# All four blocks of the second batch form their up-projection from seven products

## The chip, the cores and the metric

The kernel runs on one core of a Trainium2 chip. The metric is the time of one execution in microseconds (us) on the device. Before the change it is 642.26 us, the median of three runs (642.01 to 642.44).

## What is computed

Three layers follow each other. Only the first feed-forward layer matters here.

```python
# attention: 2 batches x 8 heads, 576 positions, head size 64
x = (pooled attention repeated 4 times) + (attention in a band of +-3 positions)
x = x.transpose(0, 2, 1, 3).reshape(1152, 512)
# layer 1: 512 -> 2048 -> 512
h = x @ w_in
g = where(h > 0, h, exp(min(h, 0)) - 1)        # ELU
x = g @ w_out
# layer 2: 4 experts of 512 -> 1024 -> 512 with gates from domain_probs
```

Every float32 matrix product is made of three products on TensorE: each operand is split into a rounded part ("hi") and the rest ("lo"), and hi x hi, hi x lo and lo x hi are added up in PSUM. A split costs one copy on ScalarE (hi) and one subtraction (lo), on GpSimd for weights and on VectorE for activations.

## The kernel before

**Order of the work.** Attention goes by pairs of heads, u = 0 to 7; pairs 0 to 3 belong to batch 0, pairs 4 to 7 to batch 1. Layer 1 goes by blocks of 512 of the 2048 hidden units, four for each batch, numbered w = 0 to 7. Each engine has its own program, written out by hand, and waits on semaphores of the others. Nothing is reordered.

Blocks w = 0 to 3 (batch 0) are "mixed": `mixed_block1` runs 16 groups g of 12 matmuls with 288 columns (8 up-projections, 8 down-projections), and between them attention for pair u = w + 4 of batch 1. VectorE's `add_outputs` puts the output of the pair into `y_acc` (the raw x of batch 1), after the y addition of group 14. ScalarE's and VectorE's `split_x` then make `x_hi` and `x_lo` of it, in group 15.

Block w = 4, the first of batch 1, is plain: 16 groups of 12 matmuls, of which the first two are opened by `open_groups` in an order that starts with the x chunks that are ready first.

Blocks w = 5 to 7 are `block7`. Their up-projection is a 2 x 2 block product formed from seven products instead of eight (Winograd's form of Strassen's scheme): 7 x 2 x 6 = 84 matmuls, and 96 for the down-projection. The products stand in this order on TensorE, two PSUM banks each (p = 0, 1): P1 (weights and tokens as they are), P6 (weight sum S2 by token sum T2), P2, P5 (S1 by T1), P7 (tokens of the quadrant that T3 replaced), P4 (by T4), P3 (S4). They are joined by VectorE's `sum_u2`, `sum_w`, `sum_c22`, `sum_c21` and `sum_c12`; P4 waits for `sum_c22`, since it adds onto a bank that `sum_c22` reads. Between these sums lies the ELU of each finished part: ScalarE `exp_part` (Relu, Exp), VectorE `max_part`, ScalarE `hi_part`, VectorE `lo_part`.

**The token sums** T1 to T4 of batch 1 are made once: raw by VectorE's `add_x`, hi by ScalarE's `xt_hi`, lo by VectorE's `xt_lo`. Before the change this lies beside the 16 groups of the plain block w = 4. **The weight sums** of a block are made once for each block: raw by GpSimd's `add_ws` (4 instructions), hi by ScalarE's `split_ws`, lo by GpSimd's `split_ws` (7 instructions with the plain weights); for w = 5 this lies beside the plain block too.

Of the kernel before, what the change touches and what calls it, by code (L numbers as in the profile page):

```python
# [14 lines left out]
FACTOR = 4  # L15
# [47 lines left out]
BLOCKS7 = 3  # L63
# [14 lines left out]
T2_, T1_, T4_, T3_ = range(4)  # L78
T_RAW = (0, 1, 3)
# [11 lines left out]
OPEN = (4, 2)  # L91
# [21 lines left out]
def program(nc, q, k, v, w_in, w_out, probs, w1, w2, out):  # L113
# [12 lines left out]
    with ExitStack() as ctx:  # L126
# [30 lines left out]
        def input_set(spare):  # L157
# [6 lines left out]
        own_set = (sb1("q_in", [LT, NLT, 2 * HD])[:], sb1("k_in", [LT, NLT, 2 * HD])[:],  # L164
                   sb1("v_in", [PT, 4, FACTOR * HD])[:], sb1("v_win", [2 * WIN, CHUNKS, 2, HD])[:])
# [18 lines left out]
        x_sum = sb1("x_sum", [128, SEQ])  # L184
# [33 lines left out]
        def xt_raw(t):  # L218

            return h_spare2[:, t, 0:SEQ].rearrange("p (k n) -> p k n", k=2)  # L220
# [174 lines left out]
        def _(pe):  # L395
# [189 lines left out]
            def mixed_block1(i, u):  # L585

                for g in range(GROUPS1):
                    if not isinstance(i, int) or g >= OPEN[0]:
# [23 lines left out]
            def block7(w):  # L612
# [251 lines left out]
        def _(act):  # L864
# [67 lines left out]
            def group1(w, b, g, between=(), next_wa=True, this_wb=True):  # L932
                if g < UP1:
                    elu_parts(w, g)
                for step, *where in between:
                    step(*where)
                if 1 <= g <= UP1:
                    elu_hi(w, b, g - 1)
                if this_wb and g < FC - 1:
                    split_wb(w, g)  # L940
                if this_wb and g == FC - 2:
                    split_wb(w, FC - 1)
                if next_wa and g >= UP1 and g < UP1 + KC:
                    split_wa(w + 1, g - UP1, groups_before1(w) + UP1)

            def split_ws(w, n):

                v = w - FIRST7
                raw = s_raw1 if isinstance(w, int) and w < 2 * BLOCKS1 else s_raw
                act.wait_ge(wa_loaded, 16 * (w + 1))  # L950
                if n in (0, 1, 3, 4):
                    c = n if n < 2 else n - 1
                    act.wait_ge(s_raw_ready, 4 * v + 3)
                    nc.scalar.copy(wa_hi[:, c, :], wa_raw[:, c, :]).then_inc(wa_hi_ready, 1)  # L954
                else:
                    q = {2: S2, 5: S1, 6: S4}[n]
                    act.wait_ge(s_raw_ready, 4 * v + 4 if q == S4 else 4 * v + 3)
                    nc.scalar.copy(s_hi[:, q], raw[:, q]).then_inc(s_hi_ready, 1)

            def xt_hi(t):  # L960

                act.wait_ge(xt_raw_ready, {T1_: 1, T3_: 2, T2_: 3, T4_: 4}[t])
# [3 lines left out]
            def block7(w):  # L966
# [186 lines left out]
            for g in range(UP1 + 1):
                group1(BLOCKS1, 1, g, next_wa=False)
            split_ws(FIRST7, 0)
            split_ws(FIRST7, 1)
            split_ws(FIRST7, 2)
            xt_hi(T2_)
            split_ws(FIRST7, 3)
            split_ws(FIRST7, 4)  # L1160
            xt_hi(T1_)
            split_ws(FIRST7, 5)
            split_ws(FIRST7, 6)
            xt_hi(T4_)
            xt_hi(T3_)
            block7(FIRST7)
# [13 lines left out]
        def _(dve):  # L1180
# [109 lines left out]
            def add_x():  # L1290

                dve.wait_ge(out_free, OUT_CREDIT + 2 * PAIRS)
                nc.vector.tensor_tensor(xt_raw(T1_), x_quad(0, 1), x_quad(0, 0), ALU.subtract).then_inc(xt_raw_ready, 1)
                nc.vector.tensor_tensor(xt_raw(T3_), x_quad(1, 1), x_quad(0, 1), ALU.subtract).then_inc(xt_raw_ready, 1)
                dve.wait_ge(xt_raw_ready, 1)
                nc.vector.tensor_tensor(xt_raw(T2_), x_quad(1, 1), xt_raw(T1_), ALU.subtract).then_inc(xt_raw_ready, 1)
                dve.wait_ge(xt_raw_ready, 3)
                nc.vector.tensor_tensor(xt_raw(T4_), x_quad(1, 0), xt_raw(T2_), ALU.subtract).then_inc(xt_raw_ready, 1)
# [8 lines left out]
            def block7(w, beside):  # L1307
# [244 lines left out]
            add_x()
            lows = {12: [(xt_lo, 1, T2_)], 13: [(xt_lo, 2, T1_)], 14: [(xt_lo, 3, T4_)], 15: [(xt_lo, 4, T3_)]}
            for g in range(GROUPS1):
                group1(BLOCKS1, 1, g, lows.get(g, ()), first=True)
# [5 lines left out]
            block7(FIRST7, token_sums)  # L1561
# [21 lines left out]
            block7(FIRST7 + 1, gates_and_zeros)  # L1583
# [7 lines left out]
            block7(FIRST7 + 2, last_zeros)  # L1591
# [12 lines left out]
        def _(pool):  # L1604
            def sum_v(u):
# [3 lines left out]
                if not isinstance(u, int):  # L1609
# [113 lines left out]
            with pool.Fori(0, BLOCKS1) as i:  # L1723
# [13 lines left out]
            split_y(0, range(3))  # L1737
# [3 lines left out]
            split_ws(FIRST7 + 2, s_raw1)  # L1741
            split_y(0, range(3, Y_PARTS))
# [36 lines left out]
```

## Time and profile before

| | |
|---|---|
| median of the runs | 642.26 us |
| the profiled execution | 643.81 us |
| its span (first to last instruction) | 642.0 us |
| TensorE busy | 632.8 us (99%) |
| VectorE, ScalarE, GpSimd busy | 349.4, 283.4, 322.6 us |
| granted TensorE clock | 1.0 of full speed |

The chain that ended last is 94% TensorE, 3% VectorE, 2% ScalarE and 1% DMA. Rows below name engines as PE (TensorE matmul), PEld (its weight load), DVE (VectorE), ACT (ScalarE), POOL (GpSimd). A matmul is issued while the one before still drains, so rows of a matmul overlap: the step from start to start is its price, not its duration. The same holds, less strongly, for the other engines.

### The profile page before, as it was taken

Reading aid. Unit: us, or ns where it says so; the run is one execution under the profiler, and the core shown is the slowest. Engines: PE = TensorE matmul, PEld = TensorE weight load, DVE = VectorE, ACT = ScalarE, POOL = GpSimd, SP = SyncE. Lnnn points to the kernel's source line nnn. Section 1 sums busy time; section 2 is a strip of 40 time slices with the busy share of each in tenths; the row PEclk is TensorE's granted clock in tenths of the full one; section 3 lists DMA queues with packets and bytes.
Section 4 is the critical chain, followed back from the end, with each engine's and each line's share of the span. In section 5 each row is a group of like instructions: output and inputs, shape, how many; then the busy total and the mean of one; then the engine's idle time right before and its main releaser. Section 6 shows DMA issues by size and latency. Waiting matters only on the chain.

```text
span 642.0 us, 13095 instructions
## 1 busy us (share of the span) xinstructions
PE 632.8 (99%) x4775; PEld 584.8 (91%) x4775; DVE 349.4 (54%) x764; ACT 283.4 (44%) x786; POOL 322.6 (50%) x278
## 2 busy tenths in 40 slices
PE   8989999999999999999999999999999999999997
PEld 5779999999999999999899899899899899989986
DVE  4977454555567787673454364355265355355352
ACT  4888474747558578453152062152152142242210
POOL 3684545454497999887247056065064164160200
PEclk9999999999999999999999999999999999999999
DMA  9974525142241123103022021011012022020012
GB/s 169 185 195 135 137 72 141 65 105 65 67 131 67 65 80 117 66 27 107 0 58 75 2 65 65 0 65 65 0 65 65 0 65 65 0 66 2 0 50 98
DMA packets 51491, 46.10 MB, mean 72 GB/s; under 512 B 31616, under 2 KB 33920, under 8 KB 51456
## 3 DMA queue, kind: packets, MB, share of 16 engines
q1 hardware_dynamic: 50272, 45.34, 25.4%
q8 instruction: 21, 0.34, 0.2%
q10 hardware_dynamic: 1184, 0.30, 0.2%
q14 instruction: 14, 0.11, 0.1%
HBM read 43.27 MB, written 2.36 MB: 71 GB/s over the span
## 4 chain that ended last, share of the span: by engine, by line
PE 94%; DVE 3%; ACT 2%; DMA 1%; issue 0%; SPq 0%
PE psum L533 16%; PE psum L534 16%; PE psum L535 16%; PE psum L604 11%; PE psum L608 11%; PE psum L606 11%; PE psum L674 2%; PE psum L672 2%; PE psum L673 2%; PE psum L462 1%; DVE neg_max L1216 1%; PE psum L439 1%; DMA q_in<-in_q 1%; PE psum L525 1%; ACT attn L884 1%; PE psum L579 1%
## 5 line engine op out<-in xcount | busy, mean ns | idle before, releaser
L1630 POOL TENSOR_TENSOR wb_lo<-wb_raw,wb_hi 128x512 fp32r<-128x512 f32 x64 | 81.8, 1297 | 179.9 <-ACT wb_hi L913 179.7
L1440 DVE SCALAR_TENSOR_TENSOR o_acc<-psum,gate_now,o_acc 128x512 f32<-128x512 f32 x72 | 54.0, 751 | 126.0 <-PE psum L535 125.7
L535 PE MATMUL psum<-wb_hi,h_lo 128*128 128x512 f32 x288 | 112.3, 390 | 0.0
L534 PE MATMUL psum<-wb_lo,h_hi 128*128 128x512 f32 x288 | 112.2, 390 | 0.0
L533 PE MATMUL psum<-wb_hi,h_hi 128*128 128x512 f32 x288 | 112.0, 389 | 0.0
L1023 ACT ACTIVATE h_hi<-psum 128x320 fp32r<-128x320 f32 (+1 forms) x128 | 52.5, 412 | 87.3 <-DVE psum L1412 40.3
L1630 POOL TENSOR_TENSOR wa_lo<-wa_raw,wa_hi 128x512 fp32r<-128x512 f32 x60 | 77.5, 1317 | 16.8 <-ACT wa_hi L954 16.8
L1029 ACT COPY sums<-psum 128x256 f32<-128x256 f32 (+1 forms) x32 | 12.8, 400 | 155.1 <-PE psum L608 155.1
L608 PE MATMUL psum<-x_hi,wa_lo 128*128 128x256 f32 (+2 forms) x228 | 67.4, 296 | 0.0
L606 PE MATMUL psum<-x_lo,wa_hi 128*128 128x256 f32 (+2 forms) x228 | 67.3, 295 | 0.0
L604 PE MATMUL psum<-x_hi,wa_hi 128*128 128x256 f32 (+2 forms) x228 | 67.2, 295 | 0.0
L535 PEld LDWEIGHTS psum<-wb_hi,h_lo 128*128 128x128 f32 x288 | 54.1, 188 | 11.3
L1394 DVE SCALAR_TENSOR_TENSOR h_lo<-psum,h_hi 128x320 fp32r<-128x320 f32 (+1 forms) x128 | 54.9, 450 | 17.1 <-ACT h_hi L1023 17.0
L533 PEld LDWEIGHTS psum<-wb_hi,h_hi 128*128 128x128 f32 x288 | 54.1, 188 | 10.9
L534 PEld LDWEIGHTS psum<-wb_lo,h_hi 128*128 128x128 f32 x288 | 54.1, 188 | 10.8
L533 PE MATMUL psum<-h_hi,wb_hi 128*128 128x288 f32 x160 | 48.9, 306 | 0.1
L534 PE MATMUL psum<-h_lo,wb_hi 128*128 128x288 f32 x160 | 47.1, 294 | 0.0
L535 PE MATMUL psum<-h_hi,wb_lo 128*128 128x288 f32 x160 | 47.1, 294 | 0.0
L606 PE MATMUL psum<-t_lo,s_hi 128*128 128x320 f32 (+2 forms) x152 | 44.9, 295 | 0.0
L608 PE MATMUL psum<-t_hi,s_lo 128*128 128x320 f32 (+2 forms) x152 | 44.8, 295 | 0.0
L604 PE MATMUL psum<-t_hi,s_hi 128*128 128x320 f32 (+2 forms) x152 | 44.8, 295 | 0.0
L604 PEld LDWEIGHTS psum<-x_hi,wa_hi 128*128 128x128 f32 x228 | 43.0, 189 | 0.6
(192 smaller groups left out, 1667.1 us busy)
## 6 DMA issues: line engine op xcount, KB each, us to landing
wa_raw<-in_moe_w_in SPq DMA_DIRECT2D x8, 1024.0 KB, 5.3
wb_raw<-in_moe_w_out SPq DMA_DIRECT2D x8, 1024.0 KB, 5.2
wa_raw<-in_moe_w SPq DMA_DIRECT2D x8, 1024.0 KB, 5.0
wb_raw<-in_moe_w SPq DMA_DIRECT2D x8, 1024.0 KB, 5.1
out<-o_acc SPq DMA_DIRECT2D x9, 256.0 KB, 2.0
v_win<-in_v SPq DMA_DIRECT2D x20, 80.0 KB, 3.6
q_in<-in_q SPq DMA_DIRECT2D x10, 144.0 KB, 4.6
v_in<-in_v SPq DMA_DIRECT2D x5, 288.0 KB
```

The costliest lines, as they stand in the source:

```text
L533: nc.tensor.matmul(bank_cols, w_hi(n), x_hi_(n), start=(n == 0), stop=False)
L534: nc.tensor.matmul(bank_cols, w_hi(n), x_lo_(n), start=False, stop=False)
L535: last = nc.tensor.matmul(bank_cols, w_lo(n), x_hi_(n), start=False, stop=(n == chunks - 1))
L604: nc.tensor.matmul(bank, w_op[0][:, k, :], x_op[0][:, k, :], start=(start and k == 0), stop=False, skip_group_check=True)
L606: nc.tensor.matmul(bank, w_op[0][:, k, :], x_op[1][:, k, :], start=False, stop=False, skip_group_check=True)
L608: last = nc.tensor.matmul(bank, w_op[1][:, k, :], x_op[0][:, k, :], start=False, stop=(stop and k == 1), skip_group_check=True)
L672: nc.tensor.matmul(to, wb_hi[:, f, cols], h_hi[:, f, t], start=(f == 0), stop=False)
L673: nc.tensor.matmul(to, wb_hi[:, f, cols], h_lo[:, f, t], start=False, stop=False)
L1023: nc.scalar.activation(h_hi[:, 2 * fh + p, t0 + width * th:t0 + width * (th + 1)], psum[:, bank[p], 0:width], ACT.Relu).then_inc(h_hi_read ...
L1394: nc.vector.scalar_tensor_tensor(h_lo[at], bank(banks, p), 0.0, h_hi[at].bitcast(F32), ALU.max, ALU.subtract).then_inc(h_lo_ready, 1)
L1440: nc.vector.scalar_tensor_tensor(o_acc[:, m, :], psum[:, DOWN2_BANKS[(MT * half + m) % 2], :], gate_now[:, m:m + 1], o_acc[:, m, :], ALU.m ...
L1630: nc.gpsimd.tensor_tensor(lo[:, c, :], raw[:, c, :], hi[:, c, :].bitcast(F32), ALU.subtract).then_inc(lo_ready, 1)
```

## The change

`block7` now serves all four blocks of batch 1, w = 4 to 7 (`FIRST7` goes from 5 to 4). The plain block w = 4 with its `open_groups` start is gone.

- The weight sums of w = 4 are made in the last mixed block: GpSimd's `add_ws` comes behind its `split_wb(3)` and ahead of the three `normalise` of pair 7, `split_ws` behind them; ScalarE's seven `split_ws` take the place of the four `split_wa`, in groups 8 to 14.
- The token sums move too. VectorE makes T1 in group 12 of the last mixed block, the first half of T2 in group 13, the second half behind the y addition of group 15. T3, the last `x_lo` and T4 come inside block w = 4, and so do all `xt_hi` and `xt_lo`.
- The raw token sums lie in `o_acc`, `s_hi` and `s_lo` before `t_hi` and `t_lo` in memory, and waits for that are added.
- The additions into `y_acc` of w = 4 are copies, as in the plain block before. What the blocks w = 5 to 7 do beside their products stays with the same distance to the end.

```diff
-BLOCKS7 = 3
+BLOCKS7 = BLOCKS1
 # TensorE
-            for k in range(KC):
-                open_groups(BLOCKS1, 1, k, *range(OPEN[1]))
-            for g in range(OPEN[1], GROUPS1):
-                group1(BLOCKS1, 1, g)
+            pe.wait_ge(out_free, 2 * PAIRS + OUT_CREDIT)
+            pe.wait_ge(x_lo_ready, KC + 2)
             with pe.Fori(FIRST7, 2 * BLOCKS1) as w:
                 block7(w)
 # TensorE, block7, ahead of P2 and of P7, P4
+                pe.wait_ge(x_lo_ready, 2 * KC)
...
-                pe.wait_ge(xt_lo_ready, 4)
+                pe.wait_ge(xt_lo_ready, 3)
...
+                pe.wait_ge(xt_lo_ready, 4)
 # ScalarE, group1 of the last mixed block
+                if not next_wa and g >= UP1 and g < UP1 + KC + 3:
+                    split_ws(w + 1, g - UP1)
 # ScalarE, block7
+                if sums_of_x:
+                    xt_hi(T2_)
+                    xt_hi(T1_)
                 copy_p1(0)
-                split_wb(w, 0)
+                if not sums_of_x:
+                    split_wb(w, 0)
                 copy_p1(1)
+                if sums_of_x:
+                    xt_hi(T3_)
+                    xt_hi(T4_)
+                    split_wb(w, 0)
                 split_wb(w, 1)
                 split_wb(w, 2)
                 split_wb(w, 3)
                 exp_part(0, BANK_A, p2_done, 0)
 # VectorE, block7
+                if first:
+                    xt_lo(1, T2_)
+                    xt_lo(2, T1_)
+                    add_x(4)
+                    split_x(PAIRS - 1, 1, BLOCKS1 - 1)
+                    add_x(5)
                 sum_u2(0)
                 sum_u2(1)
+                if first:
+                    xt_lo(3, T3_)
                 max_part(0, BANK_A)
                 sum_w(0)
+                if first:
+                    xt_lo(4, T4_)
                 max_part(1, BANK_A)
 # VectorE, last mixed block
+                    12: [(add_x, 0)] if last else [],
+                    13: [(add_x, 2)] if last else [],
                     14: [(add_outputs, u, MIXED, i)],
-                    15: [(split_x, u, 1, i)],
+                    15: [(add_x, 3)] if last else [(split_x, u, 1, i)],
 # GpSimd
-            with pool.Fori(0, BLOCKS1) as i:
+            with pool.Fori(0, BLOCKS1 - 1) as i:
...
+            sum_v(PAIRS - 1)
+            split_wb(BLOCKS1 - 1)
             add_ws(FIRST7, s_raw1)
+            for j in range(3):
+                normalise(PAIRS - 1, j)
             split_ws(FIRST7, s_raw1)
             split_wb(FIRST7)
```

## Rows read from the trace of the kernel before

**Rows 1.** The page: busy time, share of the span, instructions of TensorE.

```profile
PE 632.8 (99%) x4775; PEld 584.8 (91%) x4775; DVE 349.4 (54%) x764; ACT 283.4 (44%) x786; POOL 322.6 (50%) x278
```

**Rows 2.** Windows, blocks w = 4 and w = 5: length, each engine's busy time, clock, DMA.

```profile
166.01:191.81 25.80, 25.70 (x194) 25.47 (x193) 16.74 (x32) 17.38 (x40) 20.08 (x15) 1.00 0.25 79
191.81:215.90 24.09, 24.09 (x183) 23.86 (x181) 19.79 (x40) 16.98 (x40) 18.67 (x14) 1.00 0.16 57
```

**Rows 3.** Timeline of TensorE (start, duration, instruction): P1, P2, P7's end, P4 of w = 5.

```profile
191.81 0.29 PE L604 MATMUL psum<-x_hi,wa_hi 128*128 128x288 f32 x1
...
194.97 0.29 PE L604 MATMUL psum<-x_hi,wa_hi 128*128 128x288 f32 x1
...
199.60 0.29 PE L608 MATMUL psum<-x_hi,wa_lo 128*128 128x288 f32 x1
199.88 0.40 PE L604 MATMUL psum<-t_hi,wa_hi 128*128 128x288 f32 x1
```

**Rows 4.** Timeline of VectorE where the last mixed block ends.

```profile
164.61 0.46 DVE L1285 TENSOR_TENSOR y_acc<-psum,y_acc 128x288 f32<-128x288 f32 x1 [2.72 <-PE psum L535]
164.98 0.81 DVE L1248 TENSOR_TENSOR y_acc<-psum,o_pooled 128x288 f32 x2
166.21 0.46 DVE L1285 TENSOR_TENSOR y_acc<-psum,y_acc 128x288 f32<-128x288 f32 x1 [0.41 <-PE psum L535]
...
167.43 0.75 DVE L1293 TENSOR_TENSOR h_spare<-y_acc 128x576 f32<-128x576 f32 x1
168.10 0.75 DVE L1294 TENSOR_TENSOR h_spare<-y_acc 128x576 f32<-128x576 f32 x1
```

**Rows 5.** Timeline of VectorE: a lo part of token sums with GpSimd busy, and idle.

```profile
189.19 1.22 DVE L1304 TENSOR_TENSOR t_lo<-h_spare,t_hi 128x576 fp32r<-128x576 f32 x1
...
192.46 0.74 DVE L1304 TENSOR_TENSOR x_lo<-h_spare,x_hi 128x576 fp32r<-128x576 f32 x1
```

**Rows 6.** Timeline of ScalarE: x split, token sums, weight splits and first ELU of w = 5.

```profile
165.94 0.68 ACT L903 CAST x_hi<-y_acc  x1 [2.81 <-DVE y_acc L1248]
...
185.80 0.67 ACT L964 CAST t_hi<-h_spare 128x576 fp32r<-128x576 f32 x1
186.38 0.67 ACT L964 CAST x_hi<-h_spare 128x576 fp32r<-128x576 f32 x1
...
193.91 1.67 ACT L913 CAST wb_hi<-wb_raw 128x512 fp32r<-128x512 f32 x3
195.96 0.41 ACT L980 ACTIVATE elu<-psum 128x288 f32<-128x288 f32 x1 [0.39 <-PE psum L608]
```

**Rows 7.** Timeline of VectorE in w = 5: `max_part(0)`, `sum_w(0)`, `max_part(1)`, `sum_c22`.

```profile
196.88 0.46 DVE L1318 SCALAR_TENSOR_TENSOR psum<-elu,psum 128x288 f32<-128x288 f32 x1 [1.25 <-ACT elu L983]
197.54 0.46 DVE L1333 TENSOR_TENSOR sums<-psum,sums 128x288 f32<-128x288 f32 x1 [0.20 <-PE psum L608]
197.92 0.45 DVE L1318 SCALAR_TENSOR_TENSOR psum<-elu,psum 128x288 f32<-128x288 f32 x1
...
199.38 1.02 DVE L1339 TENSOR_TENSOR psum<-psum,sums 128x288 f32<-128x288 f32 x2
```

**Rows 8.** Timeline of GpSimd: last mixed block, then weight sums and splits.

```profile
142.42 2.52 POOL L1630 TENSOR_TENSOR wb_lo<-wb_raw,wb_hi 128x512 fp32r<-128x512 f32 x2 [0.31 <-ACT wb_hi L913]
150.07 0.91 POOL L1625 TENSOR_TENSOR attn_p<-attn_p,recip 128x432 f32<-128x432 f32 x1 [5.14 <-DVE recip L1228]
...
156.06 0.83 POOL L1625 TENSOR_TENSOR attn<-attn,recip 128x384 f32<-128x384 f32 x1 [2.50 <-DVE recip L1228]
...
187.96 3.59 POOL L1671 TENSOR_TENSOR s_lo<-o_acc,s_hi 128x512 fp32r<-128x512 f32 x2
193.80 5.06 POOL L1630 TENSOR_TENSOR wb_lo<-wb_raw,wb_hi 128x512 fp32r<-128x512 f32 x4 [2.24 <-ACT wb_hi L913]
```

**Rows 9.** Timeline of TensorE: the turn of pair 7's pooled attention.

```profile
152.08 0.82 PE L491 MATMUL psum<-ident,attn_p 128*72 128x128 f32 x6
```

**Rows 10.** Windows: the longest idle stretch of TensorE (columns as in rows 2).

```profile
38.30:39.50 1.20, 0.02 (x1) 0.05 (x1) 0.81 (x2) 1.20 (x4) 1.17 (x2) 1.00 1.25 199
```

More of the change, by code:

```diff
@@ L78 @@
 T2_, T1_, T4_, T3_ = range(4)
+XT_RAWS = {T1_: 1, T2_: 3, T3_: 4, T4_: 5}
 T_RAW = (0, 1, 3)
@@ L90 @@
 OUT_SPLIT = HALF
-OPEN = (4, 2)
+OPEN = 4
 FILL_INPUTS, FILL_SUMS = 8, 3
@@ L162, in input_set @@
                     spare[:, win_at:win_at + CHUNKS * 2 * HD].rearrange("p (c h d) -> p c h d", h=2, d=HD))
-        own_set = (sb1("q_in", [LT, NLT, 2 * HD])[:], sb1("k_in", [LT, NLT, 2 * HD])[:],
-                   sb1("v_in", [PT, 4, FACTOR * HD])[:], sb1("v_win", [2 * WIN, CHUNKS, 2, HD])[:])
+        own_q, own_k = sb1("q_in", [LT, NLT, 2 * HD])[:], sb1("k_in", [LT, NLT, 2 * HD])[:]
+        own_v, x_sum = sb1("v_in", [PT, 4, FACTOR * HD])[:], sb1("x_sum", [128, SEQ])
+        own_set = (own_q, own_k, own_v, sb1("v_win", [2 * WIN, CHUNKS, 2, HD])[:])
         spares = (o_acc[:].rearrange("p m n -> p (m n)"), h_spare[:].rearrange("p f n -> p (f n)"),
@@ L218, in xt_raw @@
         def xt_raw(t):
-            return h_spare2[:, t, 0:SEQ].rearrange("p (k n) -> p k n", k=2)
+            at = 3 * DM + SEQ * t
+            return spares[0][:, at:at + SEQ].rearrange("p (k n) -> p k n", k=2)
         def xt_at(t):
@@ L587, in mixed_block1 @@
                 for g in range(GROUPS1):
-                    if not isinstance(i, int) or g >= OPEN[0]:
+                    if not isinstance(i, int) or g >= OPEN:
                         group1(i, 0, g)
@@ L956, in split_ws @@
                     q = {2: S2, 5: S1, 6: S4}[n]
+                    if isinstance(w, int) and w == FIRST7:
+                        act.wait_ge(q_turned, PAIRS)
+                        act.wait_ge(k_turned, PAIRS)
+                        act.wait_ge(v_sum_ready, PAIRS)
                     act.wait_ge(s_raw_ready, 4 * v + 4 if q == S4 else 4 * v + 3)
@@ L960, in xt_hi, with block7 @@
             def xt_hi(t):
-                act.wait_ge(xt_raw_ready, {T1_: 1, T3_: 2, T2_: 3, T4_: 4}[t])
+                act.wait_ge(xt_raw_ready, XT_RAWS[t])
+                if t != T3_:
+                    act.wait_ge(out_free, OUT_CREDIT + 2 * PAIRS)
                 to = x_hi if t == T3_ else t_hi
                 nc.scalar.copy(to[xt_at(t)], xt_raw(t)).then_inc(xt_hi_ready, 1)
-            def block7(w):
+            def block7(w, sums_of_x=False):
                 v = w - FIRST7
@@ L1133, in _, with mixed_block1 @@
             split_wb(0, 3)
-            def mixed_block1(i, u):
+            def mixed_block1(i, u, first=False, last=False):
                 between = {
-                    0: [] if isinstance(i, int) else [(copy_qT, u, MIXED)],
+                    0: [] if first else [(copy_qT, u, MIXED)],
                     4: [(exponentiate, u, 0, MIXED)],
@@ L1147, in mixed_block1 @@
                 for g in range(GROUPS1):
-                    group1(i, 0, g, between.get(g, ()), this_wb=not isinstance(i, int))
-            mixed_block1(0, HALF_PAIRS)
-            with act.Fori(1, BLOCKS1) as i:
+                    group1(i, 0, g, between.get(g, ()), next_wa=not last, this_wb=not first)
+            mixed_block1(0, HALF_PAIRS, first=True)
+            with act.Fori(1, BLOCKS1 - 1) as i:
                 mixed_block1(i, i + HALF_PAIRS)
[L1153 to L1166, printed above, removed]
+            mixed_block1(BLOCKS1 - 1, PAIRS - 1, last=True)
+            block7(FIRST7, sums_of_x=True)
+            block7(FIRST7 + 1)
             for n in range(3):
                 split_y(0, n)
-            block7(FIRST7 + 1)
+            block7(FIRST7 + 2)
             for n in range(3, Y_PARTS):
                 split_y(0, n)
-            block7(FIRST7 + 2)
+            block7(FIRST7 + 3)
             step2(0, 0, True)
@@ L1288, in group1, with sub_x, add_x @@
                         step(*where)
[L1290 to L1298, printed above, removed]
+            def sub_x(n, out, a, b, *waits):
+                for ready in waits:
+                    dve.wait_ge(xt_raw_ready, ready)
+                nc.vector.tensor_tensor(out, a, b, ALU.subtract).then_inc(xt_raw_ready, 1)
+            def add_x(step):
+                k = step % 2
+                if step == 0:
+                    dve.wait_ge(out_free, OUT_CREDIT + 2 * (HALF_PAIRS + 2))
+                    sub_x(1, xt_raw(T1_), x_quad(0, 1), x_quad(0, 0))
+                elif step == 2:
+                    dve.wait_ge(out_free, OUT_CREDIT + 2 * (HALF_PAIRS + 3))
+                elif step == 3:
+                    dve.wait_ge(out_free, OUT_CREDIT + 2 * PAIRS)
+                if step in (2, 3):
+                    sub_x(step, xt_raw(T2_)[:, k, :], x_quad(1, 1)[:, k, :], xt_raw(T1_)[:, k, :], 1)
+                elif step == 4:
+                    sub_x(4, xt_raw(T3_), x_quad(1, 1), x_quad(0, 1))
+                elif step == 5:
+                    sub_x(5, xt_raw(T4_), x_quad(1, 0), xt_raw(T2_), 3)
             def xt_lo(n, t):
@@ L1305, in xt_lo, with block7 @@
                                         ).then_inc(xt_lo_ready, 1)
-            def block7(w, beside):
+            def block7(w, beside, first=False):
                 v = w - FIRST7
@@ L1379, in block7 @@
                     dve.wait_ge(group_done, groups_before7(w) + g + 1)
-                    nc.vector.tensor_tensor(y_acc[at], psum[:, DOWN7_BANKS[g], 0:N1], y_acc[at], ALU.add).then_inc(y_added, 1)
+                    if first:
+                        nc.vector.tensor_copy(y_acc[at], psum[:, DOWN7_BANKS[g], 0:N1]).then_inc(y_added, 1)
+                    else:
+                        nc.vector.tensor_tensor(y_acc[at], psum[:, DOWN7_BANKS[g], 0:N1], y_acc[at], ALU.add).then_inc(y_added, 1)
                     beside(g)
@@ L1532, in _, with mixed_block1 @@
             take_kTs(HALF_PAIRS)
-            def mixed_block1(i, u):
+            def mixed_block1(i, u, first=False, last=False):
                 between = {
-                    0: [] if isinstance(i, int) else [(take_in, u)],
+                    0: [] if first else [(take_in, u)],
                     3: [(row_max, u, 0, MIXED)],
@@ L1542, in mixed_block1 @@
                     9: [(reciprocals, u, 2), (copy_attnT_p, u, MIXED)],
+                    12: [(add_x, 0)] if last else [],
+                    13: [(add_x, 2)] if last else [],
                     14: [(add_outputs, u, MIXED, i)],
-                    15: [(split_x, u, 1, i)],
+                    15: [(add_x, 3)] if last else [(split_x, u, 1, i)],
                 }
                 for g in range(GROUPS1):
-                    group1(i, 0, g, between.get(g, ()), isinstance(i, int))
-            mixed_block1(0, HALF_PAIRS)
-            with dve.Fori(1, BLOCKS1) as i:
+                    group1(i, 0, g, between.get(g, ()), first)
+            mixed_block1(0, HALF_PAIRS, first=True)
+            with dve.Fori(1, BLOCKS1 - 1) as i:
                 mixed_block1(i, i + HALF_PAIRS)
[L1552 to L1555, printed above, removed]
+            mixed_block1(BLOCKS1 - 1, PAIRS - 1, last=True)
+            block7(FIRST7, lambda g: None, first=True)
             def token_sums(g):
@@ L1559, in token_sums @@
                     add_y(0, g)
-            block7(FIRST7, token_sums)
+            block7(FIRST7 + 1, token_sums)
             def gates(n):
@@ L1589, in last_zeros @@
                     nc.vector.memset(o_acc[:, g - KC, :], 0.0).then_inc(acc_zeroed, 1)
[L1591 removed]
+            block7(FIRST7 + 3, last_zeros)
             dve.wait_ge(gate_step, 4)
@@ L1608, in sum_v @@
                 pool.wait_ge(v_loaded[held(u)], 16 * loads(u))
-                if not isinstance(u, int):
+                if not isinstance(u, int) or u >= HALF_PAIRS:
                     pool.wait_ge(mixed, u)
@@ L1736, in _ @@
             split_ws(FIRST7 + 1, s_raw1)
-            split_y(0, range(3))
             split_wb(FIRST7 + 1)
@@ L1741, in _ @@
             split_ws(FIRST7 + 2, s_raw1)
+            split_y(0, range(3))
+            split_wb(FIRST7 + 2)
+            pool.wait_ge(s_lo_ready, 9)
+            add_ws(FIRST7 + 3, s_raw1)
+            split_ws(FIRST7 + 3, s_raw1)
             split_y(0, range(3, Y_PARTS))
```

6 lines of the change are left out of this document (2 added, 4 removed).

## The prediction, made before the changed kernel was run

> **What bounds the kernel now.** I read the page first: TensorE is busy for 632.8 of 642.0 us [rows 1]. Whatever takes matmuls away gains their full price, and whatever makes TensorE wait costs in full. The second view is the table by windows, cut at the block borders [rows 2]: the plain block w = 4 takes 25.80 us, the seven-product block w = 5 takes 24.09, both at full clock. The third is TensorE's timeline [rows 3], which fixes the starts of products inside a block. The others are the timelines of VectorE, ScalarE and GpSimd around the border at 166.01 us [rows 4 to 8]; there the reader is to see how much hand-made work lies between the last attention output and the first use of its token sums. Today the plain block hides it all.
>
> **What the change removes.** 192 matmuls become 180. The window of w = 5 is 24.09 us, that of w = 4 is 25.80, so if the new block w = 4 ran like w = 5 it would save 1.71 us [rows 2]. Twelve matmuls make 1.58 of it: P1 and P6, 24 matmuls, go by from 191.81 to 194.97, 0.132 us each from start to start [rows 3]. The rest is waiting inside the plain block, which goes too.
>
> **What is moved into the last mixed block.** GpSimd's last `split_wb` part ends at 144.94 [rows 8]. `add_ws`, four instructions of the kind that costs 1.27 (5.06 for four [rows 8]), ends near 150.2; the first `normalise`, so far at 150.07, follows with 0.91 and ends near 151.1. TensorE asks for it at 152.08 [rows 9], so 0.9 us of cover is left, and I cost it at nothing. `split_ws`, seven of 1.27, starts at 156.9 behind the last `normalise` and ends at 165.7, under the 166.01 at which block w = 4 starts: nothing. ScalarE has three instructions more, of 0.53 each, in groups 10 to 14, and what it does there now (`split_wa`) is of the same kind; it has a third of its time free in w = 4 (17.38 of 25.80 busy [rows 2]), and I take it to be no fuller here: nothing. VectorE's T1 and half T2 go in groups 12 and 13, where it waits (2.72 us of idle time stand before the y addition at 164.61 alone [rows 4]): nothing. The weights of w = 5 are loaded earlier than now, so no DMA is late.
>
> **What is moved into block w = 4, and on whose path.** This is where the sum is decided. Everything from the last attention output to P4 is one chain over VectorE and ScalarE. In times of this trace:
>
> 1. VectorE's y addition of group 15 starts at 166.21 and the next instruction follows 0.37 later (164.61 to 164.98) [rows 4], so the second half of T2 starts at 166.58. No row has a subtraction of 288 columns from memory to memory; half of the 0.75 of 576 columns is 0.37, an instruction of 288 with a PSUM source takes 0.46 [rows 4]. I take 0.42: 167.00.
> 2. ScalarE makes hi of T2: 0.67 [rows 6]. A hand-over between the engines costs 0.03 (ScalarE's Exp of 0.44 starts at 196.41, its Relu at 195.96, and VectorE follows at 196.88 [rows 6, 7]) to 0.15 (165.79 to 165.94 [rows 4, 6]); I take 0.1 each way: VectorE goes on at 167.87.
> 3. VectorE has five instructions of 576 columns in a row: lo of T2, lo of T1, raw T3, `x_lo` of pair 7, raw T4. They step by 0.67 and the last takes 0.75 [rows 4], with GpSimd idle, as it is from 165.7 on: T4 is ready at 167.87 + 4 x 0.67 + 0.75 = 171.30.
> 4. ScalarE makes hi of T4 (0.58 from start to start [rows 6]) from 171.40 and then four `split_wb`, 0.52 each (three in 1.67 [rows 6]): it is free at 174.06. Only then comes the first `exp_part`. In w = 5 the four splits lie between the p1 copies and the end of P2 and hide; here P2's first bank is complete at about 171.7 (six matmuls and the 0.29 of the last), and the ELU starts 2.4 us late.
> 5. `max_part(0)` is 0.92 behind that start (196.88 less 195.96 [rows 6, 7]), then `sum_w(0)` and, new, lo of T4 follow at 0.37 each. Lo of T4 runs beside GpSimd's `split_wb(4)`, which begins at 172.5 and lasts 5.06 [rows 8]: beside a busy GpSimd this instruction takes 1.22, beside an idle one 0.74 [rows 5]. I take 1.2. From `max_part(1)` to `sum_c22(0)` it is 1.46 (197.92 to 199.38 [rows 7]) and from there to P4 0.50 (to 199.88) [rows 3, 7]. P4 starts at 174.06 + 0.92 + 0.37 + 0.37 + 1.2 + 1.46 + 0.50 = 178.88.
>
> TensorE meanwhile: P1 ends at 167.59. P6 waits for lo of T2 until 168.66 (1.07 lost). P2 waits for the last `x_lo` until 170.67 (0.43 lost). P2, P5 and P7 end at 175.41, and P4 waits for 3.5 us. These three waits are not three prices: were the first two away, the third would be longer by as much.
>
> **The sum.** P4 starts 178.88 - 166.01 = 12.87 us into the block; in w = 5 it is 199.88 - 191.81 = 8.07 [rows 3]. Behind P4 everything keeps the distances of w = 5, since ScalarE and VectorE are as far as there: 215.90 - 199.88 = 16.02 [rows 2, 3]. The new block takes 28.89 us, where the plain one takes 25.80: +3.1 us. Blocks w = 5 to 7 keep what they have. The profiled execution would go from 643.81 (span 642.0) to 646.9 (645.1); it stands 1.55 above the median of 642.26, to which I apply the same difference: **645.4 us**.
>
> **Bounds.** Shortest chain: hand-overs of 0.03 (five of them, -0.35), half T2 in 0.37 (-0.05), lo of T4 in 0.67 (-0.5): +2.2. Longest: the five VectorE instructions of step 3 at 1.22 because GpSimd's weight splits end late (its two last ones took 3.59 beside VectorE instead of 2.54 [rows 8]), +2.0 by 5 x 0.4: +5.1. GpSimd has 0.3 us to spare before the block and T2 starts 0.6 after it, so the near end is the likelier.
>
> The rows show VectorE instructions with two inputs in memory at 1.22 beside a busy GpSimd and 0.74 beside an idle one [rows 5]. The Trainium skill (GPSIMD Engine Reference, section 1, Specifications) says that the memory interface is shared and that VectorE instructions with two such inputs contend. By that rule lo of T4 pays, and the ELU and sums with a PSUM input don't; the trace agrees, since the latter hold 0.46 beside GpSimd's 5.06 us stretch [rows 7, 8]. Without the rule the sum would be 0.5 us less.
>
> **Rivals.**
> - *P4 doesn't wait (not slower).* If `sum_c22(0)` were done when P7 ends, only the waits of P6 and P2 would stay, 1.50 us, and the block would come out at -1.71 + 1.50 = -0.2: 642.1 us. It decides at P7's end, 175.4: the chain would have to be 3.5 us shorter. For it: in w = 5 P4 is late by only 0.15 us (199.60 + 0.13 to 199.88 [rows 3]). Against it: four splits and hi of T4 stand ahead of the ELU in ScalarE's program, 2.7 us that nothing there can overtake. If the T2 chain were hidden as well, the full gain would stand, 640.6 us. I give the former 0.06 and the latter 0.08, for something misread in the order.
> - *The clock falls.* TensorE would idle 3.5 us before P4. Once it idles for 1.20 us and keeps full clock [rows 10], the longest idle stretch there is, so no row bears on 3.5. If P4 and P3, 24 matmuls, ran at 1.2 instead of 2.4 GHz, that is 24 x 0.132 = 3.2 us more: 648.6 us. Chance 0.08. The Trainium skill (TensorE: Matmul & The Clock Gate, Part 1) states that an idle TensorE falls back to half clock; no run here shows it so far.
> - *The mixed block is stretched.* If the four weight sums took the 1.8 each that 3.59 for two gives [rows 8], they would end 2.1 us later, `normalise` would miss 152.08 by 1.2 and the time would be 646.6. Against it: VectorE works from PSUM in that stretch. Chance 0.04.
>
> **How the numbers follow.** The forecast has 0.74 and its own range is 644.4 to 646.9. With the outer cases in part, 643.9 to 647.3 holds 8 in 10. What can be told from no change is about 0.2%, 1.3 us. Faster: 0.08 and a little for the unforeseen, 0.10. Same: 0.06. Slower: 0.84.
>
> **What would show it.** In the changed profile: GpSimd's weight sums at 145 to 150 and its splits done by 166, with the mixed block no longer; TensorE waiting about 1.1 us before P6, 0.4 before P2, and 3.5 before P4, there put down to `sum_c22`; ScalarE's four `wb_hi` copies directly ahead of the first `elu` of the block; a window of 28.9 us, followed by three of 24.1. A P4 wait under 1.5 us would make the prediction wrong, as would a faster total.

## The result and the profile after

The changed kernel takes 647.93 us (median of 6 runs, 646.18 to 648.82) where the kernel before takes 642.35 (6 runs). The ratio of the runs is 1.0070, with a 95% interval of 1.0052 to 1.0089; it makes 642.35 x 1.007 = 646.8. The medians lie 5.6 us apart, the ratio gives 4.5. It is slower, as forecast, and by more than the 3.1 us forecast. The profiled execution took 648.76 us (span 647.0).

The windows of its blocks w = 4 and w = 5 and, between them, of P4 and P3 of w = 4 (columns as in [rows 2]):

```profile
165.15:196.55 31.40, 27.33 (x182) 26.67 (x182) 19.66 (x42) 18.33 (x42) 19.36 (x15) 0.89 0.23 72
177.93:183.82 5.89, 5.89 (x25) 5.89 (x25) 4.24 (x11) 4.72 (x13) 4.16 (x4) 0.50 0.58 178
196.55:220.71 24.16, 24.07 (x182) 23.87 (x181) 18.80 (x38) 16.99 (x40) 18.70 (x14) 1.00 0.20 66
```

Block w = 4 takes 31.40 us, against 25.80 before [rows 2] and 28.89 forecast. P4 and P3, 24 matmuls, ran at a granted clock of 0.50, the lower of its two levels (1.2 GHz). What TensorE waited for between 100 and 300 us (who waits, for whom, us in total, times, longest):

```profile
PE psum L606 <- DVE psum L1359: 3.1, 1, 3.1
PE psum L606 <- DVE t_lo L1324: 0.8, 1, 0.8
PE psum L535 <- DVE h_lo L1275: 0.3, 1, 0.3
PE psum L606 <- issue: 0.2, 1, 0.2
```

The first is P4 behind `sum_c22` (3.5 forecast), the second P6 behind lo of T2. The last, for which the profile names no releaser, is P2, which needs the last `x_lo`. The third was not forecast; it lies in the last mixed block. TensorE's timeline shows the three starts, and the step behind P4:

```profile
165.15 0.39 PE L606 MATMUL psum<-x_hi,wa_hi 128*128 128x288 f32 x1
...
167.80 0.40 PE L606 MATMUL psum<-t_hi,s_hi 128*128 128x288 f32 x1 [0.81 <-DVE t_lo L1324]
...
169.80 0.39 PE L606 MATMUL psum<-x_hi,wa_hi 128*128 128x288 f32 x1 [0.16 <-issue]
...
174.54 0.29 PE L610 MATMUL psum<-x_hi,wa_lo 128*128 128x288 f32 x1
177.93 0.58 PE L606 MATMUL psum<-t_hi,wa_hi 128*128 128x288 f32 x1 [3.10 <-DVE psum L1359]
178.30 0.44 PE L608 MATMUL psum<-t_lo,wa_hi 128*128 128x288 f32 x1
178.54 0.44 PE L610 MATMUL psum<-t_hi,wa_lo 128*128 128x288 f32 x1
```

P4 starts 177.93 - 165.15 = 12.78 us into the block; the forecast was 12.87. Behind it the step is 0.24 us where it was 0.132. ScalarE's and VectorE's side of the chain, to be read beside [rows 6, 7]:

```profile
170.27 0.67 ACT L974 CAST t_hi<-o_acc 128x576 fp32r<-128x576 f32 x1 [0.66 <-DVE o_acc L1301]
170.85 2.18 ACT L915 CAST wb_hi<-wb_raw 128x512 fp32r<-128x512 f32 x4
172.93 0.40 ACT L990 ACTIVATE elu<-psum 128x288 f32<-128x288 f32 x1
```

```profile
173.84 0.46 DVE L1338 SCALAR_TENSOR_TENSOR psum<-elu,psum 128x288 f32<-128x288 f32 x1 [2.21 <-ACT elu L993]
174.21 0.45 DVE L1353 TENSOR_TENSOR sums<-psum,sums 128x288 f32<-128x288 f32 x1
174.58 1.36 DVE L1324 TENSOR_TENSOR t_lo<-o_acc,t_hi 128x576 fp32r<-128x576 f32 x1
175.87 0.45 DVE L1338 SCALAR_TENSOR_TENSOR psum<-elu,psum 128x288 f32<-128x288 f32 x1
...
177.33 0.82 DVE L1359 TENSOR_TENSOR psum<-psum,sums 128x288 f32<-128x288 f32 x2
```

Hi of T4 and four splits stand ahead of the first ELU part. VectorE idles 2.21 us for that part, and lo of T4 takes 1.36 us, since GpSimd is busy at the time; with GpSimd idle it takes 0.75 (e3).

The unforecast wait: in the last mixed block the small addition of `reciprocals(7, 0)`, 128 x 3 elements, takes 0.57 us on VectorE while GpSimd adds weights. Before the change it took 0.16, with GpSimd idle. First the changed kernel, VectorE and the GpSimd instruction beside it, then the kernel before:

```profile
148.24 0.57 DVE L1233 TENSOR_SCALAR sums<-sums 128x3 f32<-128x3 f32 x1
148.85 0.18 DVE L1235 RECIPROCAL recip<-sums 128x3 f32<-128x3 f32 x1
148.94 0.43 DVE L1275 TENSOR_TENSOR h_lo<-psum,h_hi 128x288 fp32r<-128x288 f32 x1
```

```profile
147.50 1.28 POOL L1697 TENSOR_TENSOR o_acc<-wa_raw,o_acc 128x512 f32<-128x512 f32 x1
```

```profile
149.62 0.16 DVE L1226 TENSOR_SCALAR sums<-sums 128x3 f32<-128x3 f32 x1
```

The small addition ends at 148.81, 0.03 us behind GpSimd's weight sum (147.50 + 1.28 = 148.78). The kernel before already had such cases elsewhere, for instance:

```profile
31.53 0.72 DVE L1226 TENSOR_SCALAR sums<-sums 128x3 f32<-128x3 f32 x1
```

```profile
31.40 0.83 POOL L1625 TENSOR_TENSOR attn<-attn,recip 128x384 f32<-128x384 f32 x1 [0.33 <-DVE recip L1228]
```

Again VectorE's instruction ends as GpSimd's does, at 32.25 and 32.23.

### The profile page after: what moved, and what is told of

Its sections match the earlier page's. It is cut to its first block, busy times and chain, and to the rows that moved or that the text cites. A ratio compares the mean times of both kernels' runs of the same rounds, so it can differ in the third digit from the quotient of the medians.

```text
span 647.0 us, 13072 instructions
## 1 busy us (share of the span) xinstructions
PE 633.1 (98%) x4763; PEld 585.1 (90%) x4763; DVE 354.4 (55%) x775; ACT 285.9 (44%) x791; POOL 330.8 (51%) x285
## 4 chain that ended last, share of the span: by engine, by line
PE 91%; SPq 4%; DVE 2%; ACT 1%; DMA 1%; issue 1%; DVEq 0%
PE psum L535 15%; PE psum L536 15%; PE psum L537 15%; PE psum L606 11%; PE psum L608 11%; PE psum L610 11%; PE psum L678 3%; PE psum L676 3%; PE psum L677 3%; SPq L330 2%; SPq L319 1%; SPq L315 1%; DMA wa_raw<-in_moe_w_in 1%; SPq L326 1%; PE psum L527 1%
## 5 line engine op out<-in xcount | busy, mean ns | idle before, releaser
L1047 ACT COPY sums<-psum 128x256 f32<-128x256 f32 (+1 forms) x32 | 12.8, 399 | 155.2 <-PE psum L610 155.2
L606 PE MATMUL psum<-x_hi,wa_hi 128*128 128x256 f32 (+2 forms) x240 | 71.1, 296 | 0.2 <-issue 0.2
L610 PE MATMUL psum<-x_hi,wa_lo 128*128 128x256 f32 (+2 forms) x240 | 71.0, 296 | 0.0
L608 PE MATMUL psum<-x_lo,wa_hi 128*128 128x256 f32 (+2 forms) x240 | 70.8, 295 | 0.0
L606 PE MATMUL psum<-t_hi,s_hi 128*128 128x256 f32 (+2 forms) x160 | 47.3, 296 | 0.8 <-DVE t_lo L1324 0.8
L608 PE MATMUL psum<-t_lo,s_hi 128*128 128x256 f32 (+2 forms) x160 | 47.3, 296 | 0.0
L610 PE MATMUL psum<-t_hi,s_lo 128*128 128x256 f32 (+2 forms) x160 | 47.2, 295 | 0.0
L606 PEld LDWEIGHTS psum<-x_hi,wa_hi 128*128 128x128 f32 x240 | 45.3, 189 | 1.2 <-issue 0.6
L608 PEld LDWEIGHTS psum<-x_lo,wa_hi 128*128 128x128 f32 x240 | 45.3, 189 | 0.5
L610 PEld LDWEIGHTS psum<-x_hi,wa_lo 128*128 128x128 f32 x240 | 45.3, 189 | 0.0
L535 PE MATMUL psum<-h_hi,wb_hi 128*128 128x288 f32 x128 | 39.5, 309 | 0.5 <-DVE h_lo L1275 0.3
```

Source lines behind the costliest of these rows:

```text
L535: nc.tensor.matmul(bank_cols, w_hi(n), x_hi_(n), start=(n == 0), stop=False)
L606: nc.tensor.matmul(bank, w_op[0][:, k, :], x_op[0][:, k, :], start=(start and k == 0), stop=False, skip_group_check=True)
L608: nc.tensor.matmul(bank, w_op[0][:, k, :], x_op[1][:, k, :], start=False, stop=False, skip_group_check=True)
L610: last = nc.tensor.matmul(bank, w_op[1][:, k, :], x_op[0][:, k, :], start=False, stop=(stop and k == 1), skip_group_check=True)
```

## The experiments

Times are medians of five to twelve runs, with the lowest and highest or the 95% interval of the ratio to the kernel before, measured beside them on the same chip. The length of block w = 4 in the profiled execution (P1 of w = 4 to P1 of w = 5) is the sharper measure, since the attention ahead of it varies by some 1.4 us from run to run.

**e1: the changed kernel again.** No edit.

> The changed kernel, unaltered, beside the others of this group. Theory (stall plus clock): P4 of block w = 4 starts 12.8 us into the block in every run; where the granted clock then falls, the 24 matmuls of P4 and P3 step by 0.24 instead of 0.132 and the run takes 2.6 us more, 648.0 to 648.8; where it stays, 645.4 to 646.2. So the runs scatter over 645.4 to 648.8 while those of the kernel before stay within 0.5. Rival (the slow clock is a single accident of the profiled execution): the runs stay within 1 us of each other.

647.78 us (645.98 to 649.04), ratio 1.0072 [1.0052, 1.0091]. P4 starts at 12.77. The six runs had a mean granted clock of 1.0 (645.98, 646.19), 0.997 (647.07) and 0.995 (648.49 to 649.04), so the scatter goes with the clock, and the rival (all within 1 us) falls. The kernel before did not stay within the 0.5 us that was expected: its 17 runs took 641.91 to 645.18. In the profile of e1 the clock falls later than in the first one: the first matmuls of P4 go by at full step, then 14 step by 0.24. The windows of the block, of P4 with P3, and of a stretch of attention:

```profile
166.56:196.84 30.28, 26.22 (x181) 25.56 (x181) 19.51 (x42) 18.16 (x42) 19.36 (x15) 0.94 0.21 77
179.33:184.12 4.79, 4.79 (x24) 4.79 (x25) 3.69 (x10) 4.15 (x12) 4.19 (x4) 0.64 0.63 219
30.00:45.00 15.00, 12.39 (x178) 10.62 (x178) 10.73 (x23) 11.51 (x38) 11.64 (x12) 0.89 0.76 203
```

The clock was low between 30 and 45 us as well, so a run's mean clock doesn't tell where it fell.

**e2: the wait before P4 filled with matmuls that nobody needs.** `block7` gets a parameter `first`, and w = 4 stands ahead of the loop over w, as in all kernels below that treat it apart on TensorE (e5, e8 to e10).

```diff
+                if first:
+                    for _ in range(22):
+                        nc.tensor.matmul(psum[:, 6, 0:N1], wa_hi[:, 0, 0:128], x_hi[:, 2, 0:N1], start=True, stop=True)
                 pe.wait_ge(xt_lo_ready, 4)
```

> TensorE gets 22 extra matmuls of 288 columns between P7 and P4 of block w = 4, into a bank that nobody reads; they take 22 x 0.132 = 2.9 of the 3.4 us that it waits. Theory: they cost nothing, since P4 starts when VectorE's sum_c22 is there, 12.8 us into the block as before, and the clock now never falls: P4 and P3 step by 0.132, the block takes 28.9 us, the time is 645.4 +- 0.5 with little scatter. Rival 1 (the slow clock has nothing to do with the idle stretch): the slow stretch is still there, 648. Rival 2 (TensorE's own work, not the chain, sets P4): 2.9 us more, 651.

TensorE's timeline, the 22 and P4 behind them, and the windows of the block and of P4 with P3:

```profile
176.01 3.06 PE L664 MATMUL psum<-x_hi,wa_hi 128*128 128x288 f32 x22
```

```profile
166.55:195.41 28.86, 27.47 (x204) 26.83 (x203) 19.32 (x42) 18.08 (x42) 19.22 (x15) 1.00 0.19 66
179.43:182.69 3.26, 3.26 (x24) 3.26 (x25) 2.67 (x8) 3.13 (x10) 3.10 (x4) 1.00 0.73 262
```

22 extra matmuls cost next to nothing: P4 at 12.88, 0.1 us later, and the block at 28.86, which is the forecast length. P4 and P3 take 3.26 instead of 5.89 us, so the fall of the clock cost 2.63 there. In the block both rivals fall. The total doesn't show it: the median is 647.36 (645.77 to 647.73, ratio 1.0061 [1.0043, 1.0080]), 0.4 below e1, with overlapping intervals, and 2 us above the 645.4 expected. Of the five runs none lies over 648, but two took 647.36 and 647.38 with a mean clock of 1.0, which this theory doesn't explain. In the profiled one the clock was at 0.89 far ahead of this edit, in the attention:

```profile
30.00:45.00 15.00, 12.15 (x175) 10.33 (x172) 9.52 (x20) 10.65 (x38) 10.56 (x12) 0.89 0.81 198
```

This fall comes behind TensorE's wait for `x_sum`, the raw x of batch 0, ahead of the first up-projections. The end of that wait in the first profile of the changed kernel, where the clock stayed, and in e2:

```profile
38.12 0.37 PE L581 MATMUL psum<-x_hi,wa_hi 128*128 128x288 f32 x1 [1.37 <-DVE x_sum L1255]
```

```profile
38.13 0.38 PE L581 MATMUL psum<-x_hi,wa_hi 128*128 128x288 f32 x1 [1.75 <-DVE x_sum L1259]
```

The wait was 1.51 to 1.75 us in the four profiled executions with a fall there (e1, e2, e9, e10) and 1.23 to 1.37 in the other eight. Nothing was tried on it, so that the wait causes this fall is not shown.

**e3: the four weight splits behind the first ELU parts.**

```diff
-                    split_wb(w, 0)
-                split_wb(w, 1)
-                split_wb(w, 2)
-                split_wb(w, 3)
+                else:
+                    split_wb(w, 1)
+                    split_wb(w, 2)
+                    split_wb(w, 3)
                 exp_part(0, BANK_A, p2_done, 0)
                 exp_part(1, BANK_A, p2_done, 0)
                 hi_part(0, 0, 0, BANK_A)
+                if sums_of_x:
+                    split_wb(w, 0)
                 hi_part(1, 0, 0, BANK_A)
+                if sums_of_x:
+                    split_wb(w, 1)
+                    split_wb(w, 2)
+                    split_wb(w, 3)
```

> ScalarE's four splits of the down-projection weights of w = 4 come behind the first two ELU parts instead of ahead of them. Theory: the ELU starts when P2's first bank is complete, 2.0 us earlier; GpSimd is then idle while VectorE makes lo of T4, which takes 0.75 instead of 1.36; P4 starts 2.6 us earlier, waits about 0.7, the clock stays: 645.4 - 2.6 = 642.8 us. Rival (the token sums alone hold P4, and the splits hide anyway): P4 at 12.8 and 645 to 648 as before. A cost may come back at the down-projection, which needs the splits' lo parts 3.2 us behind P4: up to 0.5 us.

643.84 us (643.32 to 647.77), ratio 1.0026 [1.0011, 1.0041], 3.9 less than e1. P4 starts at 10.43, 2.35 earlier. On ScalarE the ELU now starts directly behind hi of T4:

```profile
170.28 0.67 ACT L974 CAST t_hi<-o_acc 128x576 fp32r<-128x576 f32 x1 [0.66 <-DVE o_acc L1307]
170.90 0.41 ACT L990 ACTIVATE elu<-psum 128x288 f32<-128x288 f32 x1
```

The ELU starts 2.04 us earlier in the block (5.74 instead of 7.78), and the rest of the 2.35 comes with the shorter lo of T4. The block takes 26.53 us at full clock. The theory holds, and the rival (the splits hide anyway) falls: the order of ScalarE's program put the largest piece onto the chain. The total is 1.0 us above the 642.8 expected, which was counted from 645.4, while the changed kernel took 646.0 to 646.2 in three of its four runs with a mean clock of 1.0.

**e4: lo of T4 in VectorE's idle time ahead of `max_part(0)`.** `xt_lo(4, T4_)` moves up two lines.

> VectorE makes lo of T4 ahead of max_part(0), in the 2.2 us in which it waits for ScalarE, instead of between sum_w(0) and max_part(1). Theory: the chain to P4 is 1.3 us shorter (1.36 and its hand-over), P4 waits about 2.1 us, at 11.5 us into the block, and the clock stays with a shorter idle stretch: 645.4 - 1.3 = 644.1 us. Rival (lo of T4 lies beside other work): no difference from the changed kernel.

P4 at 11.53, block 27.52: 1.3 us less than 28.86, as expected. The total does not show the gain: it is 646.02 (645.07 to 647.94, ratio 1.0066 [1.0047, 1.0086]), 1.9 above the 644.1 expected. Of five runs, two near 647.9 have a mean clock of 0.995 and 0.994, and of the three at 1.0 (645.07, 645.99, 646.02) only one lies below the 645.98 of e1. The profiled one, with a wait of 1.9 us before P4, kept full clock in the block; where it fell in the two others no profile shows. Lo of T4 takes 0.75 here although GpSimd's splits start with it; it is they that take longer, 5.63 us instead of 5.06 [rows 8].

**e5: T1 first and P5 ahead of P6.** VectorE's `xt_lo` change places in the same way. The edit, cut to ScalarE:

```diff
-                    xt_hi(T2_)
                     xt_hi(T1_)
+                    xt_hi(T2_)
...
```

> The changed kernel with T1's hi and lo ahead of T2's and TensorE's products of w = 4 in the order P1 P5 P6 P2 P7 P4 P3; nothing else moves. T1's raw sum is there early, so P5 starts where P6 waited, and the waits of 1.1 and 0.4 us ahead of P6 and P2 go. Theory (the three waits are one chain): P4 starts 12.8 us into the block all the same, behind a wait of 4.8 us instead of 3.4; nothing is gained, and with a longer idle stretch the clock falls in more of the runs: 646 to 649. Rival (each wait has its own price): 1.5 us less than the changed kernel in runs of the same clock, P4 at 11.3.

The windows of the block and of P4 with P3, and TensorE's waits:

```profile
166.48:197.43 30.95, 26.58 (x182) 26.14 (x181) 20.24 (x42) 18.35 (x42) 19.82 (x15) 0.89 0.22 77
179.21:184.70 5.49, 5.49 (x24) 5.49 (x25) 3.85 (x11) 4.34 (x12) 4.16 (x4) 0.55 0.60 191
```

```profile
PE psum L606 <- DVE psum L1393: 4.2, 1, 4.2
PE psum L535 <- DVE h_lo L1309: 0.3, 1, 0.3
PE psum L606 <- DVE t_lo L1358: 0.2, 1, 0.2
```

TensorE's products of w = 4 stand in the order P1 P5 P6 P2 P7 P4 P3. P4 stays at 179.21 - 166.48 = 12.73 although 1.1 us of waiting ahead of it went: the waits are one chain, and the last took over what the first lost (4.2 instead of 3.1; 4.8 was expected). The rival (P4 at 11.3) falls. 648.64 us (647.18 to 651.50), ratio 1.0083 [1.0053, 1.0112].

**e6: both moves**, the edits of e3 and e4 together.

> Both moves together: the four weight splits behind the first ELU parts, and lo of T4 ahead of max_part(0). Theory: the ELU starts when P2's first bank is complete, so VectorE's gap is gone and T3's and T4's lo parts push max_part(0) by 0.4; P4's wait is 0.4 us where it is 1.05 with the splits alone; 0.6 us less than that kernel, the clock never falls: 643.2. Rival (the moves add up to 2.4 + 1.3): P4 wouldn't wait at all, 642.2.

P4 at 9.83, block 26.47, 0.06 less than e3 and not 0.6. P4's own wait fell to 0.2, but the splits' lo parts come too late for the down-projection now, with a wait of 0.4 on GpSimd's `wb_lo`: P4 and P3 take 3.81 us to it instead of 3.28. 644.93 us (643.39 to 648.10), ratio 1.0027 [1.0008, 1.0045], where 643.2 was expected. The size expected was wrong: what was gained at P4 was lost 3.8 us later. "The clock never falls" was wrong too: two of the twelve runs, 647.70 and 648.10, have a mean clock of 0.994 and 0.995.

**e7: the fourth weight sum behind `normalise(7, 0)`**, on top of e6.

```diff
-            add_ws(FIRST7, s_raw1)
-            for j in range(3):
-                normalise(PAIRS - 1, j)
+            add_ws(FIRST7, s_raw1, parts=(0, 1, 2))
+            normalise(PAIRS - 1, 0)
+            add_ws(FIRST7, s_raw1, parts=(3,))
+            normalise(PAIRS - 1, 1)
+            normalise(PAIRS - 1, 2)
```

> As the kernel with both moves, and GpSimd's fourth weight sum comes behind normalise(7, 0). In the profile of the changed kernel VectorE's small addition in reciprocals(7, 0), 128 x 3 elements, takes 0.57 instead of 0.16 us while GpSimd adds weights, lo of h follows late, and TensorE waits 0.35 us at group 8 of the last mixed block. Theory (the shared memory interface holds it): beside an idle GpSimd it takes 0.16 again, the wait goes, 0.4 us less: 642.8. Rival (the unrolled last block itself costs it): 0.57 and the wait stay.

VectorE's addition, and GpSimd's `normalise` behind it, ahead of which GpSimd idles for 1.27 us:

```profile
147.78 0.16 DVE L1239 TENSOR_SCALAR sums<-sums 128x3 f32<-128x3 f32 x1
```

```profile
148.22 0.91 POOL L1664 TENSOR_TENSOR attn_p<-attn_p,recip 128x432 f32<-128x432 f32 x1 [1.27 <-DVE recip L1241]
```

0.16 again, TensorE's wait at group 8 is gone, and block w = 4 starts at 164.27 instead of 164.72 (e6): shown. The unrolled last block, the rival, is still there and costs nothing. 643.36 us (642.99 to 646.44), ratio 1.0013 [0.9997, 1.0030], where 642.8 was expected.

**e8: products in the order P1 P5 P2 P6 P7 P4 P3**, with VectorE's work in a matching order, on top of e7.

> The attempt at a version that beats both: as the one before, with T1 first, products P1 P5 P2 P6 P7 P4 P3, the last x_lo second, both sum_w early, T4's lo last before sum_c22. Theory: only 0.2 us of waiting ahead of P5, none ahead of P2 and P6, P4 about 9.0 us into the block instead of 9.9: 642.0, level with the kernel before or 0.3 under it. Rival (VectorE's hand-made work still sets P4 whatever the order): P4 stays at 9.8 and above, 642.8.

P4 at 175.97 - 165.84 = 10.13, block 26.12: the rival was right, and the theory (P4 at 9.0, 642.0 us) wrong. VectorE works without a gap from 166.9 us to `sum_c22`. 644.14 us (642.40 to 644.41), ratio 1.0010 [0.9996, 1.0024].

**e9: lo of T4 before GpSimd's splits begin**, on top of e8.

> As the reordered kernel, with lo of T4 directly behind lo of T3 and sum_u2(0), before GpSimd's weight splits begin. In the reordered kernel VectorE works without a gap from 166.9 us to P4 and lo of T4 takes 1.28 there beside a busy GpSimd. Theory (VectorE's work is the bound of that stretch): it takes 0.75, P4 starts 0.5 us earlier, 9.6 us into the block instead of 10.1, the block takes 25.6 us (the plain one took 25.8). Rival (something else sets P4): 10.1 and 26.1 as before.

Lo of T4 took 0.75, yet P4 starts at 177.76 - 167.83 = 9.93 and the block takes 26.63. `sum_u2(1)` now comes behind it, so the second half of P7 waits (0.6), and `wb_lo` is late for the down-projection (0.4). 643.94 us (643.19 to 647.64), ratio 1.0011 [0.9996, 1.0027]. The expected P4 at 9.6 and block of 25.6 us did not come: 0.2 us came off P4 and 0.7 went elsewhere.

**e10: five wait instructions less for TensorE in each of w = 5 to 7**, on top of e9: the waits on `xt_lo_ready` (4) and `x_lo_ready` (1) stand in w = 4 alone.

> As the one before, and TensorE's waits for the x and token sums, which matter in w = 4 alone, are gone from the loop over w = 5 to 7. In the changed kernel P4 of these blocks is 8.17 us behind P1 instead of 8.07, and the only difference is one more wait instruction ahead of it. Theory (each wait instruction there costs about 0.1 us while TensorE's data are just ready): 8.07 again or less, three times 0.1 us, 24.09 us for each block. Rival (what VectorE does sets it): 8.17 and 24.16 stay.

The start of P4 in w = 5 of this kernel, and the window of that block:

```profile
200.51 0.40 PE L606 MATMUL psum<-t_hi,wa_hi 128*128 128x288 f32 x1
```

```profile
192.43:216.53 24.10, 24.10 (x182) 23.87 (x181) 18.85 (x38) 16.98 (x40) 19.80 (x15) 1.00 0.28 87
```

P4 is 8.08 behind P1 (8.16 in e9, 8.17 in the changed kernel, 8.07 before) and the block takes 24.10 (24.15, 24.16, 24.09). So the waits do cost it, and the rival falls. The theory's price of 0.1 us for each wait instruction doesn't hold: all five together gave 0.08 at P4. The kernel before, with three of the five, has P4 at 8.07, and e10, with none, at 8.08, so by this comparison the two added ones cost; which of the two, no run tells. It is worth 0.05 us a block, below what the runs can tell: 644.25 us (642.93 to 646.34), ratio 1.0015 [1.0000, 1.0030]. No version beat the kernel before; e7 to e9 can't be told from it.

## Why the prediction was right, and where its sizes were not

The direction and the mechanism, a chain over VectorE and ScalarE that holds P4, were right. The size was too small: the median of 647.93 lies 0.6 us above the top of the range of 643.9 to 647.3, and 646.8, which the ratio gives, lies inside it. The range itself stopped short of its own outer cases, the longest chain (642.26 + 5.1 = 647.4) and the fall of the clock (648.6).

- **The chain sets P4, and its length.** Forecast 12.87 us into the block, measured 12.78, 12.77 and, with the wait filled, 12.88. Step by step, with the block's start taken as zero: half of T2 starts at 0.46 (forecast 0.57), raw T4 is done at 5.08 (5.29), the first ELU part starts at 7.78 (8.05), lo of T4 takes 1.36 (1.2). Shown by e3 and e4, which take a link out each: P4 starts 2.35 and 1.3 us earlier.
- **Three waits are not three prices.** Shown by e5: without the wait ahead of P6, the one ahead of P4 is 4.2 instead of 3.1 us, and P4 starts where it did.
- **The block at full clock: 28.89 forecast, 28.86 measured (e2).** So 28.86 - 25.80 = 3.06 us of the loss is the forecast mechanism.
- **The clock.** The forecast held it at full speed and gave the fall 0.08 as a rival, at 3.2 us. It fell in the profiled executions of the changed kernel, of e1 and of e5, with waits of 3.1, 3.1 and 4.2 us before P4; it did not fall in w = 4 in the seven with 1.9 us or less, nor in e2, where the wait was filled. It cost 2.6 us in the first (5.89 less 3.26) and 1.4 in e1 (30.28 less 28.86). The 3.2 us of the rival took the step to double, to 0.264; it went to 0.24. This term was left out of the likeliest case. Runs with a mean clock of 0.997 or less are more frequent where the wait is long: in the comparison of e1 to e4 they are 4 of 6 in e1 and 2 of 5 in e4, but 1 of 5 in e2, 1 of 11 in e3 and 1 of 17 of the kernel before. That the fall before P4 is what lifts the median from some 646 to 647.9 is nevertheless not shown: e2, without it, has 647.36. The Trainium skill (TensorE: Matmul & The Clock Gate, Part 1) states that an idle stretch sends TensorE back to 1.2 GHz; the trace agrees, with 0.50 in P4 and P3. The rival deserved more than 0.08 for a wait forecast at 3.5 us, when the longest one that had been seen, and had kept the clock, was 1.20 us.
- **The weight sums in the mixed block were costed at nothing**, since `normalise` has 0.9 us of cover. That step failed on another path: not through a late `normalise`, which came in time, nor through slower weight sums (they took 1.28 to 1.29 us each, and the rival had 1.8), but through VectorE's small addition, 0.41 us late behind GpSimd, and 0.35 us of waiting at group 8. The rival on that stretch was argued away with "VectorE works from PSUM in that stretch"; the small addition doesn't, and the trace of before showed what happens to it (31.53 us, 0.72 instead of 0.16). Shown by e7.
- **"Blocks w = 5 to 7 keep what they have"**: 24.16 instead of 24.09, by the two wait instructions that the change added (e10).

Together 3.06 + 0.35 + 3 x 0.07 = 3.6 us without a fall of the clock. Runs of the changed kernel at a mean clock of 1.0 took 645.98, 646.18, 646.19 and 647.62; three of them are 3.6 to 3.8 over 642.35. The 647.62 is not explained. With the 2.6 of the clock the sum is 642.35 + 6.2 = 648.6, where the profiled execution has 648.76, but that is luck in part. From profile to profile (span 642.0 and 647.0) block w = 4 is 5.60 us longer and the three behind it 0.2, while w = 4 starts 0.86 earlier (165.15 and 166.01); and that start lies between 165.15 and 166.56 in two executions of the same changed kernel, so 0.35 us there can be read only where its wait stands.

## What to carry to other kernels

Work that a plain stage hides has to be placed anew when that stage goes: 12 matmuls less saved 1.6 us and uncovered a chain of 12.8 us, whose largest avoidable link (2.0 us) was only the order of ScalarE's program. Add up such a chain across the engines from the last input to the first product that needs it; several waits along it are one price, best found by its last member. And a long wait on TensorE may cost more than its length: one of 3.1 us cost 2.6 us more in one profiled execution and 1.4 more in another, through the clock behind it.

## What the runs showed of the hardware

- A VectorE instruction of 128 x 3 elements, with a single tensor input in memory, took 0.57 instead of 0.16 us beside a busy GpSimd. What it lost doesn't go by its own size but by what GpSimd still had to do. In the kernel before, in its first 180 us, seven such instructions begin while one of GpSimd runs: six took 0.27 to 1.28 us, and each ended 0.02 to 0.03 us behind GpSimd's; the seventh began 0.03 us before GpSimd's end and took 0.17.
- 22 matmuls placed into a wait of 3.1 us cost 0.1 us, and in the profiled execution the products behind them ran at full clock.
- The clock falls in other places too: it was 0.89 from 30 to 45 us in e1 and e2, behind a wait of 1.51 and 1.75 us. A wait of 1.9 us in another place (e4, before P4) kept it. Of the 23 runs of the kernel before in one comparison (that of e9 and e10), 7 had a mean clock of 0.997 or less; they took 643.62 to 645.77 us, where the fastest took 642.20.
